# Loading w_out's quarters between w_in's, starting the first projections on half of the mixed weights, and turning the combination's weights in the rounded format

## The reference

```python
# attention over q, k, v -> x of 2304 tokens x 512 (window of 128, slopes per head, softmax)
logits = x @ phi                                   # 2304 x 32
slot_input = softmax(logits, over tokens).T @ x    # 32 x 512
for e in range(8):                                 # 4 slots each
    slot_out[e] = relu(slot_input[e] @ w1[e]) @ w2[e]
c = softmax(logits, over slots)                    # 2304 x 32, "the combination's weights"
x = c @ slot_out                                   # 2304 x 512
h = relu(x @ w_in)                                 # w_in 512 x 2048
out = (h * h) @ w_out                              # w_out 2048 x 512
```

## Time and profile before

| | us |
|---|---|
| time of three runs: median (lowest to highest) | 403.23 (402.55 to 403.57) |
| time of the profiled execution | 402.54 |
| its span | 400.7 |
| TensorE busy | 388.4 (97%) |
| VectorE busy | 283.5 (71%) |
| ScalarE busy | 264.4 (66%) |
| GpSimd busy | 97.9 (24%) |

### The profile page before, as it was taken

The page is one execution under the profiler, slowest core; times in us unless marked ns, Lnnn a source line. Parts: engine busy times, 40 slices in busy tenths (PEclk is TensorE's granted clock), DMA queues, the critical chain, the costliest instruction groups (busy, mean ns, idle before and its releaser), DMA issues.

```text
span 400.7 us, 8879 instructions
## 1 busy us (share of the span) xinstructions
PE 388.4 (97%) x3316; PEld 320.1 (80%) x3316; DVE 283.5 (71%) x741; ACT 264.4 (66%) x609; POOL 97.9 (24%) x94
## 2 busy tenths in 40 slices
PE   7699999999999999999899999999999999999997
PEld 6478888787877654444578888889999999999996
DVE  5788888888872655023899994658786978777752
ACT  4989899898972421001875877858877767777720
POOL 4687777868661010000053000000000000000000
PEclk9999999999999999999999999999999999999999
DMA  6688899989698479999900101001010101001011
GB/s 193 174 304 252 250 319 245 311 252 262 191 290 284 150 272 334 404 386 386 374 7 1 54 0 52 2 0 54 0 55 2 54 0 52 0 0 52 2 52 54
DMA packets 50021, 61.39 MB, mean 153 GB/s; under 512 B 25536, under 2 KB 33728, under 8 KB 48320
## 3 DMA queue, kind: packets, MB, share of 16 engines
q1 hardware_dynamic: 49440, 60.37, 45.3%
q10 hardware_dynamic: 544, 0.52, 0.4%
HBM read 56.16 MB, written 4.72 MB: 152 GB/s over the span
## 4 chain that ended last, share of the span: by engine, by line
PE 84%; DVE 5%; ACT 4%; DMA 4%; issue 1%; POOL 1%; SPq 1%; POOLq 0%; DVEq 0%
PE psum L1597 9%; PE psum L1598 9%; PE psum L1599 9%; PE psum L1315 6%; PE psum L1271 6%; PE psum L1297 6%; PE psum L1571 4%; PE psum L1572 4%; PE psum L1573 4%; DMA win_sb<-in_moe_w_in 4%; PE psum L1472 3%; PE psum L1583 3%; PE psum L1493 2%; PE psum L1230 2%; PE psum L1383 2%; ACT probs L1004 2%
## 5 line engine op out<-in xcount | busy, mean ns | idle before, releaser
L897 DVE TENSOR_TENSOR step_lo<-step_raw,step_hi 128x896 fp32r<-128x896 f32 x48 | 50.2, 1088 | 25.5 <-ACT step_hi L1140 25.4
L1004 ACT ACTIVATE probs<-probs,row_min 128x256 f32<-128x256 f32 (+1 forms) x128 | 60.0, 471 | 12.0 <-DVE row_min L642 12.0
L584 POOL TENSOR_TENSOR probs<-probs,row_inv 128x1024 f32<-128x1024 f32 x31 | 59.1, 1928 | 23.5 <-DVE row_inv L693 23.5
L1597 PE MATMUL psum<-t_hi,step_hi 128*128 128x256 f32 x192 | 53.8, 280 | 0.1
L1599 PE MATMUL psum<-t_hi,step_lo 128*128 128x256 f32 x192 | 53.7, 280 | 0.0
L1598 PE MATMUL psum<-t_lo,step_hi 128*128 128x256 f32 x192 | 53.7, 279 | 0.0
L1140 ACT CAST step_hi<-step_raw 128x896 fp32r<-128x896 f32 x48 | 42.8, 944 | 7.1 <-DVE step_raw L910 6.7
L1152 ACT ACTIVATE step_raw<-psum 128x512 f32<-128x512 f32 x48 | 26.0, 595 | 28.8 <-PE psum L1583 24.9
L642 DVE CUSTOM_DVE_ANT_0 probs<-psum,rel 128x256 f32<-128x256 f32 (+1 forms) x128 | 42.0, 385 | 2.9 <-PE psum L1271 2.8
L1599 PE MATMUL psum<-wout_hi,step_lo 128*128 128x256 f32 x144 | 40.3, 280 | 0.0
L1597 PE MATMUL psum<-wout_hi,step_hi 128*128 128x256 f32 x144 | 40.2, 280 | 0.0
(11 more groups left out here) (183 smaller groups left out, 858.1 us busy)
## 6 DMA issues: line engine op xcount, KB each, us to landing
ring<-in_moe_w SPq DMA_DIRECT2D x16, 1024.0 KB, 6.3
ring<-in_moe_w SPq DMA_DIRECT2D x4, 2048.0 KB, 11.8
q_raw<-in_q SPq DMA_DIRECT2D x16, 256.0 KB, 3.5
v_in<-in_v SPq DMA_DIRECT2D x32, 128.0 KB, 2.8
ring_x<-in_moe_w SPq DMA_DIRECT2D x2, 2048.0 KB, 8.3
win_sb<-in_moe_w_in SPq DMA_DIRECT2D x4, 1024.0 KB, 12.3
wout_raw<-in_moe_w_out SPq DMA_DIRECT2D x4, 1024.0 KB, 14.5
out_x<-out_sb SPq DMA_DIRECT2D x8, 512.0 KB, 2.8
```

Source lines behind the costliest of these rows:

```text
L584: nc.gpsimd.tensor_tensor(probs[:, par, h, 0:4, :], probs[:, par, h, 0:4, :], row_inv[:, par, 4 * h:4 * h + 4].unsqueeze(2).to_broadcast([ ...
L897: nc.vector.tensor_tensor(step_lo[j][:, i, 1:8, :], step_raw[j][:, i, 1:8, :], step_hi[j][:, i, :, :].bitcast(F32), ALU.subtract).then_inc ...
L1004: nc.scalar.activation(t, t, ACT.Exp, bias=row_min[:, par, one:one + 1], scale=-1.0, accum_out=row_sum[:, par, one:one + 1]).then_inc(exp_ ...
L1597: mm(to, hi, w_hi, start=clears, stop=False, skip_group_check=True)
```

## The change

**Loads.** SyncE issues win 0, win 1, wout 0, win 2, wout 1, win 3, wout 2, wout 3.

**Order of the mix and the first tile.** The mix's quarters 0 and 1 are made first; quarters 2 and 3 are made between the first projections. Each unit's split of w_out is placed beside its `low_part` and `high_part` in new places. The units that GpSimd splits stay the same.

**Transposes.** The combination's weights (`comb`) and an identity (`ident_r`) are held in fp32r, and the five turns transpose in that format. A VectorE copy makes `ident_r`. `soT` moves to another place in SBUF.

```diff
-        comb = sb("comb", [P, QT * B, 4, NS])
+        comb = sb("comb", [P, QT * B, 4, NS], F32R)
+        ident_r = sb("ident_r", [P, P], F32R)
...
-            for i in range(4):
-                load_win(i)
-            for i in range(4):
-                load_wout(i)
+            load_win(0)
+            load_win(1)
+            load_wout(0)
+            load_win(2)
+            load_wout(1)
+            load_win(3)
+            load_wout(2)
+            load_wout(3)
...
+            nc.vector.tensor_copy(ident_r[:, :], ident[:, :]).then_inc(comb_ready, 1)
```

VectorE's `first`, and its new `first_group`, which `step` calls in tile 0 in place of the loop over units 2 to 7:

```diff
             def first():
                 take_part(1)
+                split_low(0)
                 take_mix(0)
                 take_mix(1)
-                take_part(3)
                 low_part(0)
-                split_low(0)
-                take_mix(2)
                 low_part(1)
                 split_low(1)
+                low_part(2)
+
+            def first_group():
+                take_mix(2)
+                split_low(2)
+                low_part(3)
+                take_part(3)
+                low_part(4)
+                split_low(4)
+                low_part(5)
                 take_mix(3)
+                low_part(6)
+                split_low(6)
+                low_part(7)
```

ScalarE's, likewise:

```diff
             def first():
                 take_part(0)
+                split_high(0)
                 take_mix(0)
-                take_part(2)
                 take_mix(1)
                 high_part(0)
-                split_high(0)
+                high_part(1)
+                take_part(2)
+                split_high(1)
+                high_part(2)
+
+            def first_group():
+                split_high(2)
                 take_mix(2)
-                high_part(1)
-                split_high(1)
+                split_high(3)
+                high_part(3)
+                split_high(4)
+                high_part(4)
+                split_high(5)
+                high_part(5)
                 take_mix(3)
+                split_high(6)
+                high_part(6)
+                split_high(7)
+                high_part(7)
```

The five turns of transposes on TensorE (`comb_turn`):

```diff
-                    pe.wait_ge(comb_ready, 2)
+                    pe.wait_ge(comb_ready, 3)
...
-                    last = nc.tensor.transpose(psum[:, (2, 7)[t % 2], P * j:P * j + P],
-                                               comb[:, B * t + j, :, :].rearrange("p d s -> p (d s)"), ident[:, :])
+                    last = nc.tensor.transpose(psum[:, (2, 7)[t % 2], P * j:P * j + P].bitcast(F32R),
+                                               comb[:, B * t + j, :, :].rearrange("p d s -> p (d s)"), ident_r[:, :])
```

TensorE's `first` makes `mix_parts(0)`, `(1)`, `mix_sum(0)`, `(1)`, waits for `mix_ready` 1, then `hidden` of units 0 and 1, `mix_parts(2)`, and behind `mix_ready` 2 `hidden` of unit 2. Then:

```diff
             def first_step():
                 project(0, 0, 0, 0)
+                mix_sum(2)
+                hidden(0, 3, 3)
+                project(0, 1, 1, 0)
+                mix_parts(3)
                 pe.wait_ge(mix_ready, 3)
-                hidden(0, 3, 3)
                 hidden(0, 4, 4)
-                project(0, 1, 1, 0)
+                project(0, 2, 2, 0)
                 hidden(0, 5, 5)
-                project(0, 2, 2, 0)
+                mix_sum(3)
+                project(0, 3, 3, 0)
                 pe.wait_ge(mix_ready, 4)
                 hidden(0, 6, 6)
-                project(0, 3, 3, 0)
                 hidden(0, 7, 7)
+                project(0, 4, 4, 0)
                 hidden(1, 8, 0)
-                project(0, 4, 4, 0)
```

More of the change, by code:

```diff
@@ L191, in attention_moe_ffn @@
         siT = sb("siT", [P, DC, NS])
-        soT = sb("soT", [P, DC, NS])
+        ident_r = sb("ident_r", [P, P], F32R)
         assert place["at"] <= late_at
@@ L208, in attention_moe_ffn @@
         relu_h = sb("relu_h", [P, 2, 2 * FT])
+        soT = sb("soT", [P, DC, NS])
+        assert place["at"] <= late_at
         BLOCK = 4 * KH * NH
@@ L816, in _ @@
             for d in (0, 2):
-                link(nc.vector.tensor_copy(comb[:, :, d, :].bitcast(F32R), lg[:, :, :]))
+                link(nc.vector.tensor_copy(comb[:, :, d, :], lg[:, :, :]))
+            nc.vector.tensor_copy(ident_r[:, :], ident[:, :]).then_inc(comb_ready, 1)
             take_hidT(1)
             for d in (0, 2):
-                nc.vector.tensor_tensor(comb[:, :, 1 + d, :], lg[:, :, :], comb[:, :, d, :], ALU.subtract
+                nc.vector.tensor_tensor(comb[:, :, 1 + d, :], lg[:, :, :], comb[:, :, d, :].bitcast(F32), ALU.subtract
                                         ).then_inc(comb_ready, 1)
@@ L962, in step @@
                         m = FU * n + AHEAD + u
[L963 to L968, removed]
-                            low_part(m)
[L970 to L974, removed]
+                        if m == AHEAD:
+                            first_group()
+                        elif FU <= m < FU * CONV:
+                            low_part(m)
+                        elif m >= FU * CONV and AHEAD_STEPS[u] is not None:
                             next_steps(CONV, AHEAD_STEPS[u])
@@ L1657, in first @@
                 mix_sum(0)
-                mix_parts(2)
                 mix_sum(1)
-                mix_parts(3)
                 pe.wait_ge(mix_ready, 1)
                 hidden(0, 0, 0)
-                mix_sum(2)
                 hidden(0, 1, 1)
-                mix_sum(3)
+                mix_parts(2)
                 pe.wait_ge(mix_ready, 2)
@@ L1712 @@
 TURN_BANKS = (1, 0)
-MIX_BANKS = ((6, 7), (0, 4), (2, 3), (6, 7))
+MIX_BANKS = ((6, 7), (0, 4), (6, 7), (6, 7))
 LOWS_OF_POOL = (3, 5, 7)
```

## The result

The changed kernel takes 408.81 us (median of 4 runs, 406.48 to 411.01) against 403.4 for the kernel before (median of 4, 402.55 to 407.18). The ratio is 1.0117, 95% interval 1.0074 to 1.0159: slower, and by more than forecast (405.4, range 403.3 to 407.0). Measured once more beside other kernels it is 1.0104 (1.0068 to 1.014). The four runs' mean TensorE clocks are 1.00 for the fastest (406.48), 0.992, 0.992, and 0.987 for the slowest (411.01).

A forecast was written before the change was run, and what follows sets the result against it. The prediction took the chain of waits as the bound, with TensorE's own work 84% of the span. Its terms, +2.4 + 0 + 0 us on a mean of 402.97, gave 405.4 us, range 403.3 to 407.0.

The forecast's parts named there:

- the two waits: TensorE waits 1.5 to 2 us ahead of `hidden(0)` and about 2.5 us ahead of `hidden(6)`.
- Part 1: Up to the first projection: casts wait for w_out's first quarter at 188.4; `project(0)` starts at 194.0, 2.2 us early.
- Part 2: TensorE from `project(0)` to `project(3)`: the 2.2 us lead pays for three moved mix pieces, 2.9 us; 0.35 us left.
- Part 3: VectorE up to `take_mix(3)`: GpSimd's holds of 2.2 us end it at 211.1; `hidden(6)` waits 2.5 us.
- Later still: Rival, chance 0.11: third load 1 to 2 us late, or TensorE's clock falls in the waits; +3.4 to +5.5 us.
- the walk: Step-by-step timing of the engines through the rewritten stretch; gave +2.4 us, with 1.6 to 3.3 as its error.
- Part 4: The five turns' transposes in fp32r: counted as 0, since ScalarE then waits longer for the load at 188.4.
- The early start pays: Rival, chance 0.07: no hold and w_out's quarter 1 us earlier make it faster, -0.9 us; 400.3 to 402.1.
- The holds do not add up: Rival, chance 0.15: VectorE between split 2 and `take_mix(3)` loses less to GpSimd; not slower, 403.0 to 403.5.

The follow-up runs named there:

- kernel before without GpSimd: The kernel before with VectorE splitting w_out's units 3, 5 and 7 in place of GpSimd: 403.41 us, ratio 0.9996.
- kernel with all repairs: Changed kernel with unit 0's split behind the mix's first quarters, take_mix(3) ahead of unit 4's split, all units split by VectorE: 403.09 us, ratio 0.999.
- kernel kept at work: Changed kernel with 16 and 14 identity transposes added, so TensorE works through most of its two long waits: 406.61 us, ratio 1.0073.
- changed, no GpSimd: Changed kernel with VectorE splitting w_out's units 3, 5 and 7 in place of GpSimd: 404.38 us, ratio 1.0022.
- loads-alone kernel: The kernel before with the eight loads in the changed order, nothing else: 412.26 us, ratio 1.0196.

## Why the prediction was wrong

The direction and the two waits were right. The price was not: +2.4 us were forecast and 5.4 measured (6.0 in the profiled execution), because the falls of the clock were left out of the sum.

- **Part 1** put `hidden(0)` at 191.4 and `project(0)` at 194.0; they came at 192.3 and 195.5. The cause of the wait was the one named. w_out's quarter landed at 189.2 instead of 188.4, 0.8 us late: all loads from the second on were some 0.9 us later than in the profile before, and so they are in the profile of the kernel before without GpSimd, where w_in's third quarter lands 14.7 us behind the start of the last expert's products against 13.8. So executions scatter by this much without the change; in the five profiles of the changed order in which ScalarE waits for this quarter it lands 14.1 to 14.8 us behind the same point, and whether the new order has a share in that is not shown. The range of the landing was given as 0.5.
- **Part 2** (the lead pays for three moved pieces) was right, and shown by the kernel with all repairs: at best level with before.
- **Part 3** was right in what decides: two holds, squares of 2.88 and 2.89 us, a wait of 2.62 us where 2.5 was forecast. `take_mix(3)` ended at 213.2 instead of 211.1, 2.1 us late, of which 1.8 were there at `mix_sum(2)` (198.62 instead of 196.8).
- **The step that failed** is the clock, which stands in the prediction only as one of two causes of "Later still", with 0.11: "Against: 1.46 us at 196.24 with the clock at 1.00 in its surroundings". A wait of 1.46 us was taken to speak for one of 2.5. The rows that could tell were not there: behind the first 3 us no wait of TensorE in the trace before is longer than 1.60 us. The clock fell at both. Its price here: `mix_parts(2)`, `hidden(2)` and the start of `project(0)` late by 0.9 us net at `mix_sum(2)` (198.62 - 192.31 = 6.3 us behind `hidden(0)`, against 5.4 in the walk and 5.5 in the kernel kept at work), and 1.6 us at the second place, where 3.4 us of dense work ran at half (218.18 - 213.27 = 4.9 us from `hidden(6)` to `hidden(8)`, against 3.3 in the kernel kept at work). 2.4 + 0.8 + 0.9 + 1.6 = 5.7 of the 6.0 us.
- Without the falls the sum was nearly right: the two executions of the changed kernel with a mean clock of 1.00 took 406.48 and 406.29 us and the eight kept at work 406.37 in the median, 3.0 us above the kernel before, against 2.4 forecast with 1.6 to 3.3 as the walk's error. 402.97 + 2.4 + 0.8, for the late quarter, is 406.2.
- **Part 4** was right: 0, shown by the transposes alone.
- **The rivals.** "Later still" came true, mainly by the clock; its other cause, the third quarter 1 to 2 us late, is there with 0.8 us. Its upper end was 408.5; the medians are 408.81 and 408.38. "The early start pays" is excluded by the kernel with all repairs. "The holds do not add up" fell with the two rows of 2.88 and 2.89.

## What to carry to other kernels

A wait of TensorE is not priced by its length alone: where a change turns several short waits into one long one, ask what the clock was behind the longest wait of the trace, and if there is none as long, put its fall into the sum's range and not into a rival of 1 in 10. When an order is written by hand, look at what stands ahead of the instruction that another engine waits for; moving one `take_mix` by two places took back half of the loss or more. Two engines that hold each other up can cost more than one doing both jobs: 2.2 us of hold against 1.14 of own work. And before a fall of the clock is put down to a change, look whether the kernel before has it too, in some executions: here 16 of 84 have a mean clock below 1.00.

## What the runs showed of the hardware

- From the mix on, TensorE's clock fell to half around the end of waits of 2.62, 2.75, 2.76, 2.77 and 3.30 us in seven profiles, from 0.6 us ahead of the wait's end to 1.1 us behind it, for 3.4 us in most and for 6.8 us in one (changed, no GpSimd: 0.58 and 0.74 in the 10 us from 195), and for 6.8 us from within the wait of 7.17 us. At one wait of 2.67 us (the first of the loads-alone kernel) it did not fall, nor at any of 1.5 us or less. In two of nine executions of the changed kernel the mean clock was 1.00 with the same order, so a wait of this length makes the fall likely and not certain.
- A shorter wait is not always safe. Near 18 us TensorE waits 1.60 us in every profile, behind a wait of 1.05 to 1.08 us some 3 us earlier; in five of fourteen the clock fell there, for 6.8 us.
- A GpSimd instruction that waits under a VectorE split runs before VectorE's next square, in every such row of the ten profiles that have one (202.18 before, 201.29 and 216.37 after), and ends 2.24 to 2.27 us behind that split.
- Four fp32r transposes of 128 columns cost 0.12 us less than four in f32 (0.37 against 0.49 from the turn's start to the next product).
